# A fused attention and two-MLP kernel: its MLP products as seven block products over thirds of the tokens, with the output product between the gate's and the value's

## The chip, the cores and the metric

The kernel runs on one core of a Trainium2 chip. The metric is the device time of one execution in microseconds. The engines are TensorE (PE, matrix products, with its weight loads as PEld), VectorE (DVE), ScalarE (ACT), GpSimd (POOL) and SyncE (SP), whose queue issues the DMAs here. Each engine works through its own queue of instructions in order; semaphores hold one engine for another. PSUM, which TensorE writes, has eight banks of 512 float32 columns in each of 128 partitions.

## The reference

Windowed attention with a distance bias (4 batches of 576 tokens, 8 heads of 64, window 128), then a gated MLP, then a product of two linear maps with two more matrices. T is 2304 tokens, the model width 512.

```python
scores = where((rel >= 0) & (rel < 128), q @ k.T / 8 - slope[h] * rel, -1e9)
x = softmax(scores) @ v                                   # (2304, 512)
x = (sigmoid(x @ w_gate) * (x @ w_val)) @ w_out           # d_ff 1536
y = ((x @ w1) * (x @ w2)) @ w3 @ w_out2                   # d_ff 1024
```

## The kernel before

All products are made in three passes of float32r: every operand is split into a high part (a cast, `*_hi`) and a rest (`*_lo`, the difference), and `product` (lines 371 to 376) issues hi x hi, lo x hi and hi x lo into the same bank. So each tensor that TensorE reads costs other engines a cast and a subtraction.

**Attention.** 16 pairs of heads in 5 steps each give 80 steps; each engine has a function `slot` that works on several steps at once, with lags between scores (TensorE), `score` (VectorE, line 671), exponentials (ScalarE), `reciprocals` (VectorE, 682 and 684), `normalise` (GpSimd, 852), `turn` (TensorE), the split of the turned probabilities (ScalarE 560, VectorE 691) and `pv` (TensorE). The result is written twice: ScalarE casts it to `x_hi` (567), VectorE subtracts to `x_lo` (`out_lo`, 699). In the same slots TensorE multiplies w3 with the second output matrix (`fold`), 8 blocks in 8 steps, so that the second MLP has one matrix less; VectorE and GpSimd split w3 (646, 825).

**MLPs.** x, h and the outputs are held transposed (features in the partitions). The hidden features are taken in groups of 256: 6 groups (G1) for the first MLP, 4 (G2) for the second. In a group the tokens go by in five chunks (`CHUNKS`), four of 512 and one of 256. `stage1` makes, for a chunk and each half f of the group, the gate's bank `a_ps` and the value's bank `b_ps` from 4 blocks of x (24 matmuls a half); ScalarE makes `side` from `a_ps` (sigmoid or copy, 604), VectorE multiplies it with `b_ps` to `hid` (759), ScalarE casts `h_hi` (607) and GpSimd subtracts `h_lo` (888). `stage2` makes the four output banks `o_ps` from them, and VectorE adds each to `acc` in SBUF (769, 771). TensorE's `group` issues stage1 of the next chunk before stage2 of this one:

```python
for c in range(NCH):
    if c + 1 < NCH:
        stage1(g, c + 1, wb)
    elif more:
        stage1(g + 1, 0, 1 - wb)
    stage2(g, c, wb)
```

The next group's three weight matrices (1024 columns each) are loaded by SP (343), cast by ScalarE (597) and subtracted by GpSimd (880) once per group, into the other of two sets of buffers. At the end of the first MLP VectorE splits `acc` into the new x (780, 784). Outputs are stored from `acc` (357, 366).

## Time and profile before

| | us |
|---|---|
| median of 3 runs | 969.59 |
| the runs | 968.31, 969.59, 1548.55 |
| span of the profiled execution | 966.6 |
| TensorE busy | 937.0 |
| VectorE busy | 422.0 |
| ScalarE busy | 315.3 |
| GpSimd busy | 334.8 |

The profiled execution's own time is known as its span, from the first to the last instruction; the median of the runs is 3.0 us above it. Busy time of TensorE counts a matmul from its start to its modelled end, though the next one starts earlier, so the spacing of the starts is what a matmul costs in a row. A row of the grouped views gives a line, the engine, what is written from what, the shape and the count, then the busy time and the mean ns of one, then the engine's idle time before them and what ended it. A row of the timeline gives start and duration in us.

### The profile page before, as it was taken

What the parts mean: (1) busy time and instruction counts of PE and PEld (TensorE: products, weight loads), DVE (VectorE), ACT (ScalarE), POOL (GpSimd) and SP (SyncE); (2) the same over time, 40 slices, a digit from 0 to 9 for tenths busy, and PEclk for the clock granted to TensorE, in tenths of its full rate; (3) what the DMA queues carried; (4) which work ended last, traced back from release to release, by engine and by line L of the source; (5) the groups of instructions that cost most, each with busy time, mean ns of one, the idle gap of its engine ahead of it and who ended that gap; (6) DMA issues with size and microseconds to landing.
All of it is one profiled execution on the core that took longest, in us unless ns stands there. A gap on an engine that the chain in (4) does not pass through costs nothing.

```text
span 966.6 us, 14591 instructions
## 1 busy us (share of the span) xinstructions
PE 937.0 (97%) x4912; PEld 799.1 (83%) x4912; DVE 422.0 (44%) x1115; ACT 315.3 (33%) x819; POOL 334.8 (35%) x314
## 2 busy tenths in 40 slices
PE   5899999999999999999999999999999999999998
PEld 4788888787888888888888888888888888888887
DVE  8999999994222222232232222345322222223223
ACT  6787888774211212121222121121121111121111
POOL 7677666661331231231231241231221222322211
DMA  6333333322010010010000000000000000000022
GB/s 217 104 114 108 96 109 102 106 101 77 22 44 1 22 44 1 22 43 0 22 24 19 22 22 22 22 22 22 22 22 22 22 22 22 1 0 1 1 87 109
DMA packets 28984, 44.95 MB, mean 47 GB/s; under 512 B 2464, under 2 KB 14368, under 8 KB 28960
## 3 DMA queue, kind: packets, MB, share of 16 engines
q1 hardware_dynamic: 28960, 44.64, 14.7%
q8 instruction: 14, 0.23, 0.1%
q14 instruction: 10, 0.08, 0.0%
HBM read 37.81 MB, written 6.82 MB: 46 GB/s over the span
## 4 chain that ended last, share of the span: by engine, by line
PE 80%; DVE 13%; issue 4%; ACT 1%; DMA 0%; SPq 0%; DVEq 0%; ACTq 0%
PE a_ps L374 9%; PE o_ps L375 9%; PE a_ps L375 9%; PE o_ps L374 9%; PE b_ps L375 8%; PE b_ps L374 8%; PE o_ps L376 8%; PE b_ps L376 8%; PE a_ps L376 8%; DVE pt_lo L691 3%; DVE rowsum L682 2%; DVE x_lo L699 2%; DVE w_hi L646 2%; DVE negs L671 2%; PE pv_ps L374 1%
## 5 line engine op out<-in xcount | busy, mean ns | idle before, releaser
L888 POOL TENSOR_TENSOR h_lo<-hid,h_hi 128x512 fp32r<-128x512 f32 (+1 forms) x100 | 118.0, 1180 | 555.9 <-ACT h_hi L607 555.9
L759 DVE TENSOR_TENSOR hid<-b_ps,side 128x512 f32<-128x512 f32 (+1 forms) x100 | 63.8, 638 | 406.2 <-PE b_ps L376 404.7
L604 ACT ACTIVATE side<-a_ps 128x512 f32<-128x512 f32 (+1 forms) x100 | 55.5, 555 | 483.2 <-PE a_ps L376 483.1
L374 PE MATMUL a_ps<-x_hi,w_hi 128*128 128x512 f32 (+1 forms) x400 | 147.4, 369 | 0.3 <-DVE w_lo L748 0.3
L375 PE MATMUL o_ps<-h_lo,w_hi 128*128 128x512 f32 (+1 forms) x400 | 147.3, 368 | 0.0
L375 PE MATMUL a_ps<-x_lo,w_hi 128*128 128x512 f32 (+1 forms) x400 | 147.3, 368 | 0.0
L374 PE MATMUL o_ps<-h_hi,w_hi 128*128 128x512 f32 (+1 forms) x400 | 147.3, 368 | 0.0
L375 PE MATMUL b_ps<-x_lo,w_hi 128*128 128x512 f32 (+1 forms) x400 | 147.2, 368 | 0.0
L376 PE MATMUL b_ps<-x_hi,w_lo 128*128 128x512 f32 (+1 forms) x400 | 147.2, 368 | 0.0
L376 PE MATMUL o_ps<-h_hi,w_lo 128*128 128x512 f32 (+1 forms) x400 | 147.2, 368 | 0.0
L376 PE MATMUL a_ps<-x_hi,w_lo 128*128 128x512 f32 (+1 forms) x400 | 147.2, 368 | 0.0
L374 PE MATMUL b_ps<-x_hi,w_hi 128*128 128x512 f32 (+1 forms) x400 | 147.2, 368 | 0.0
L771 DVE TENSOR_TENSOR acc<-o_ps,acc 128x512 f32<-128x512 f32 (+1 forms) x160 | 102.1, 638 | 95.2 <-PE o_ps L376 95.0
L607 ACT CAST h_hi<-hid 128x512 fp32r<-128x512 f32 (+1 forms) x100 | 57.4, 574 | 105.7 <-DVE hid L759 105.6
L374 PEld LDWEIGHTS a_ps<-x_hi,w_hi 128*128 128x128 f32 x400 | 75.4, 189 | 13.0 <-issue 0.4
L374 PEld LDWEIGHTS o_ps<-h_hi,w_hi 128*128 128x128 f32 x400 | 75.4, 189 | 12.6
L376 PEld LDWEIGHTS a_ps<-x_hi,w_lo 128*128 128x128 f32 x400 | 75.4, 189 | 12.6
L376 PEld LDWEIGHTS o_ps<-h_hi,w_lo 128*128 128x128 f32 x400 | 75.4, 189 | 12.6
L374 PEld LDWEIGHTS b_ps<-x_hi,w_hi 128*128 128x128 f32 x400 | 75.4, 189 | 12.5
L375 PEld LDWEIGHTS o_ps<-h_lo,w_hi 128*128 128x128 f32 x400 | 75.4, 189 | 12.5
L375 PEld LDWEIGHTS b_ps<-x_lo,w_hi 128*128 128x128 f32 x400 | 75.4, 189 | 12.5
L376 PEld LDWEIGHTS b_ps<-x_hi,w_lo 128*128 128x128 f32 x400 | 75.4, 189 | 12.5
(69 smaller groups left out, 1440.9 us busy)
## 6 DMA issues: line engine op xcount, KB each, us to landing
k_raw<-kT SPq DMA_DIRECT2D x16, 288.0 KB, 2.8
q_raw<-qT SPq DMA_DIRECT2D x16, 288.0 KB, 2.8
v_raw<-v SPq DMA_DIRECT2D x16, 256.0 KB, 2.7
w_raw<-w3t SPq DMA_DIRECT2D x16, 256.0 KB, 3.1
w_raw<-w SPq DMA_DIRECT2D x8, 512.0 KB, 3.5
w_raw<-w_gate SPq DMA_DIRECT2D x6, 512.0 KB, 3.5
w_raw<-w_val SPq DMA_DIRECT2D x6, 512.0 KB, 3.5
w_raw<-w_out SPq DMA_DIRECT2D x6, 512.0 KB, 3.5
```

What stands on the lines that cost most here:

```text
L374: pe.matmul(out, lh, rh, start=start, stop=False)
L375: pe.matmul(out, lh, rl, start=False, stop=False)
L376: return pe.matmul(out, ll, rh, start=False, stop=stop)
L604: nc.scalar.activation(side[f][:, 0:n], ps_a[f][:, 0:n], func).then_inc(side_ready, 1)
L607: nc.scalar.copy(h_hi[hb][f][:, 0:n], hid[f][:, 0:n]).then_inc(h_hi_done, 1)
L646: nc.vector.tensor_copy(w3_hi[:, cols], w3_raw[:, cols]).then_inc(w3_hi_done, 1)
L671: op = nc.vector.tensor_tensor_reduce(negs[buf][:, j * KW + skip:(j + 1) * KW], pA[buf][:, first:first + KW - skip], bias[pb][:, skip:KW], ...
L682: nc.vector.tensor_scalar(rowsum2[:, cols], rowsum[:, cols], 1e-9, None, ALU.add).then_inc(sum_done, 1)
L691: nc.vector.tensor_tensor(out=cols(pt_lo[buf]), in0=cols(pB[buf]), in1=cols(pt_hi[buf]), op=ALU.subtract).then_inc(pt_split, 1)
L759: nc.vector.tensor_tensor(out=hid[f][:, 0:n], in0=ps_b[f][:, 0:n], in1=side[f][:, 0:n], op=ALU.mult).then_inc(hid_ready, 1)
L771: op = nc.vector.tensor_tensor(out=acc[:, cols], in0=ps_o[o][:, 0:size(c)], in1=acc[:, cols], op=ALU.add)
L888: nc.gpsimd.tensor_tensor(out=h_lo[hb][f][:, 0:n], in0=hid[f][:, 0:n], in1=h_hi[hb][f][:, 0:n], op=ALU.subtract).then_inc(h_split, 1)
```

## The change

The first two products of each MLP are made by a seven-product scheme on blocks of 2 x 2. The weights of a group (512 x 256) and x of some tokens (512 x 768) are cut in halves in both directions. Seven products M1 to M7 of a sum of weight blocks with a sum of x blocks, 256 x 128 by 256 x 384 each, take the place of eight block products. The tokens are taken in three passes (`NPASS`) of `TP` = 768, each through all ten groups of both MLPs; `TH` is 384.

- TensorE: `multiply(g, m, js)` makes the seven products of the gate (m = 0) or of the value (m = 1), `project(g)` the eight output tiles. Five banks hold the products (M7 is added to the bank of M4 after VectorE has read it, M6 to that of M1), three the output tiles. All loops are written out.
- ScalarE: copies M2 and M5 to `s21` and `s12`, applies the sigmoid in SBUF, casts the weights (`weights_hi`: two blocks of 512 columns in all, five sums of 1280), w_out (`out_hi`, 1024) and the hidden pieces.
- VectorE: `weight_sums` makes the five sums of weight blocks (512, 512 and 256 columns, both inputs in SBUF), `combine` makes the four quarters C21, C12, C11, C22 of the gate (in `side`) or the value (in `hid`) with six sums of 384 columns, each with one input in PSUM, `hidden` multiplies `hid` with `side`, both in SBUF, and `add_up` adds the output tiles.
- GpSimd: `weights_lo`, `out_lo` and `hidden_lo` subtract.
- Sums of x blocks (`x_sum`, 768 columns) and their splits are made before each layer of each pass, for the first in the last slots of the attention. The attention writes its result once, in float32 (`xf`), so VectorE's `out_lo` of lines 694 to 701 is gone; `xf` is overwritten by the outputs. `fold` has one block in each of 64 slots.

```diff
--- before.py
+++ after.py
-CH = 512
-CHUNKS = [slice(c, min(c + CH, T)) for c in range(0, T, CH)]
+NPASS = 3
+TP = T // NPASS
+TH = TP // 2
...
+M2, M4, M5, M3, M1, M7, M6 = range(7)
+W_S5, W_S2, W_D6, W_D7, W_S1, W_11, W_22 = range(7)
+W_OF = {M2: W_S2, M4: W_22, M5: W_S5, M3: W_11, M1: W_S1, M7: W_D7, M6: W_D6}
+BANK_OF = {M2: 0, M4: 1, M5: 2, M3: 3, M1: 4, M7: 1, M6: 4}
...
```

TensorE:

```diff
+            def multiply(g, m, js):
+                q, inst = 2 * g + m, instance(g)
+                if js[0] == M2:
+                    pe.wait_ge(wq_split[m], g + 1)
...
+                    elif j == M7:
+                        pe.wait_ge(c_done[C21], q + 1)
+                    elif j == M6:
+                        pe.wait_ge(u11_done, q + 1)
+                    for kk in range(2):
+                        w = slice(W_OF[j] * GW + kk * P, W_OF[j] * GW + (kk + 1) * P)
+                        x = slice((2 * j + kk) * TH, (2 * j + kk + 1) * TH)
+                        mm = product(quad_ps[BANK_OF[j]][:, 0:TH], (wq_hi[m][:, w], wq_lo[m][:, w]),
+                                     (xs_hi[:, x], xs_lo[:, x]),
+                                     start=kk == 0 and j not in (M7, M6), stop=kk == 1, onto=j in (M7, M6))
+                    mm.then_inc(prod_done, 1)
+            def project(g):
+                pe.wait_ge(wo_split, g + 1)
+                pe.wait_ge(h_split, 4 * (g + 1))
...
+                    wait(pe, acc_done, t - 2)
+                    for f in range(FG):
+                        w = slice(f * DM + o * P, f * DM + (o + 1) * P)
+                        hp = piece(2 * f + c)
+                        mm = product(ps_o[t % 3][:, 0:TH], (wo_hi[hb][:, w], wo_lo[hb][:, w]),
+                                     (h_hi[hb][:, hp], h_lo[hb][:, hp]), start=f == 0, stop=f == FG - 1)
+                    mm.then_inc(o_done, 1)
...
+            for g in range(NG):
+                if g == 0:
+                    multiply(0, 0, (M5, M3, M1, M7, M6))
+                else:
+                    multiply(g, 0, ALL)
+                if not first_of(g):
+                    project(g - 1)
+                multiply(g, 1, ALL)
+                if last_of(g):
+                    project(g)
-            def group(g, wb, more):
-                for c in range(NCH):
-                    if c + 1 < NCH:
-                        stage1(g, c + 1, wb)
-                    elif more:
-                        stage1(g + 1, 0, 1 - wb)
-                    stage2(g, c, wb)
```

ScalarE:

```diff
+            def weights_hi(g, m):
+                act.wait_ge(rawq_in[m], 16 * (g + 1))
+                wait(act, prod_done, 14 * g - 7 * (1 - m))
+                if g == 0:
...
+                four = raw_q[m][:, :].rearrange("p (b n) -> p b n", b=4)
+                nc.scalar.copy(wq_hi[m][:, W_11 * GW:7 * GW].rearrange("p (b n) -> p b n", b=2), four[:, 0:4:3, :]
+                               ).then_inc(wq_hi_done[m], 1)
+                act.wait_ge(wsum_done[m], 3 * (g + 1))
+                nc.scalar.copy(wq_hi[m][:, 0:5 * GW], wsum[m][:, :]).then_inc(wq_hi_done[m], 1)
...
+            for g in range(NG):
+                more = g + 1 < NG
+                keep_21(2 * g)
+                out_hi(g)
+                keep_12(2 * g)
+                sigmoid(g, C21)
+                sigmoid(g, C12)
+                keep_21(2 * g + 1)
+                sigmoid(g, C11)
+                sigmoid(g, C22)
+                keep_12(2 * g + 1)
+                if more:
+                    weights_hi(g + 1, 0)
+                for n, k in enumerate((C21, C12, C11, C22)):
+                    hidden_hi(g, n, k)
+                if more:
+                    weights_hi(g + 1, 1)
+                    if last_of(g):
+                        for j in (M2, M4, M5, M3, M1, M7, M6):
+                            xs_hi_part(instance(g) + 1, j)
```

VectorE:

```diff
+            def weight_sums(g, m):
+                dve.wait_ge(rawq_in[m], 16 * (g + 1))
+                wait(dve, wq_split[m], g)
...
+                raw, out = raw_q[m], wsum[m]
+                four = raw[:, :].rearrange("p (b n) -> p b n", b=4)
+                nc.vector.tensor_tensor(out=out[:, 0:2 * GW].rearrange("p (b n) -> p b n", b=2), in0=four[:, 0:4:2, :],
+                                        in1=four[:, 1:4:2, :], op=ALU.add).then_inc(wsum_done[m], 1)
+                nc.vector.tensor_tensor(out=out[:, 2 * GW:4 * GW], in0=raw[:, 0:2 * GW], in1=raw[:, 2 * GW:4 * GW],
+                                        op=ALU.subtract).then_inc(wsum_done[m], 1)
+                nc.vector.tensor_tensor(out=out[:, 4 * GW:5 * GW], in0=raw[:, 0:GW], in1=raw[:, 3 * GW:4 * GW],
+                                        op=ALU.add).then_inc(wsum_done[m], 1)
+            def combine(g, m):
+                q, out = 2 * g + m, (side, hid)[m]
+                if q == 0:
+                    dve.wait_ge(x_ready, NSTEP)
+                if m == 1:
+                    wait(dve, h_split, 4 * g)
+                dve.wait_ge(prod_done, 7 * q + M4 + 1)
+                dve.wait_ge(s21_done, q + 1)
+                nc.vector.tensor_tensor(out=out[:, piece(C21)], in0=quad_ps[1][:, 0:TH], in1=s21[:, :],
+                                        op=ALU.add).then_inc(c_done[C21], 1)
+                dve.wait_ge(prod_done, 7 * q + M3 + 1)
+                dve.wait_ge(s12_done, q + 1)
+                nc.vector.tensor_tensor(out=out[:, piece(C12)], in0=quad_ps[3][:, 0:TH], in1=s12[:, :],
+                                        op=ALU.add).then_inc(c_done[C12], 1)
+                wait(dve, c_done[C22], q)
+                nc.vector.tensor_tensor(out=t22[:, :], in0=quad_ps[3][:, 0:TH], in1=s21[:, :],
+                                        op=ALU.subtract).then_inc(t22_done, 1)
+                dve.wait_ge(prod_done, 7 * q + M1 + 1)
+                wait(dve, c_done[C11], q)
+                nc.vector.tensor_tensor(out=u11[:, :], in0=quad_ps[4][:, 0:TH], in1=s12[:, :],
+                                        op=ALU.subtract).then_inc(u11_done, 1)
+                if m == 1:
+                    hidden(g, 0, C21)
+                    hidden(g, 1, C12)
+                dve.wait_ge(prod_done, 7 * q + M7 + 1)
+                dve.wait_ge(u11_done, q + 1)
+                nc.vector.tensor_tensor(out=out[:, piece(C11)], in0=quad_ps[1][:, 0:TH], in1=u11[:, :],
+                                        op=ALU.add).then_inc(c_done[C11], 1)
+                dve.wait_ge(prod_done, 7 * q + M6 + 1)
+                dve.wait_ge(t22_done, q + 1)
+                nc.vector.tensor_tensor(out=out[:, piece(C22)], in0=quad_ps[4][:, 0:TH], in1=t22[:, :],
+                                        op=ALU.add).then_inc(c_done[C22], 1)
+                if m == 1:
+                    hidden(g, 2, C11)
+                    hidden(g, 3, C22)
+            def hidden(g, n, k):
+                dve.wait_ge(c_done[k], 2 * g + 2)
+                if g % GP < G1:
+                    before = 4 * (g // GP * G1 + g % GP)
+                    dve.wait_ge(sig_done, before + n + 1)
+                nc.vector.tensor_tensor(out=hid[:, piece(k)], in0=hid[:, piece(k)], in1=side[:, piece(k)],
+                                        op=ALU.mult).then_inc(hid_done, 1)
...
+            for g in range(NG):
+                more = g + 1 < NG
+                combine(g, 0)
+                if more:
+                    weight_sums(g + 1, 0)
+                if not first_of(g):
+                    add_up(g - 1)
+                combine(g, 1)
+                if more:
+                    weight_sums(g + 1, 1)
+                if last_of(g):
+                    inst = instance(g) + 1
+                    if g % GP == GP - 1:
+                        if more:
+                            for j in (M4, M3, M1, M6):
+                                x_sum(inst, j)
+                        add_up(g)
...
+                        add_up(g, range(4))
+                        x_lo_part(inst, M2)
+                        x_sum(inst, M4)
+                        add_up(g, (4, 5))
+                        x_lo_part(inst, M4)
+                        add_up(g, (6, 7))
+                        x_sum(inst, M3)
+                        x_sum(inst, M1)
+                        x_lo_part(inst, M3)
+                        x_sum(inst, M6)
+                        x_lo_part(inst, M1)
+                        x_lo_part(inst, M6)
-            def out_lo(t, s):
...
-                    op = nc.vector.tensor_tensor(out=out_cols(x_lo, t, s - 1, h), in0=pv_cols(pC[buf], i, h),
-                                                 in1=out_cols(x_hi, t, s - 1, h), op=ALU.subtract)
```

GpSimd:

```diff
+            def weights_lo(g, m):
+                pool.wait_ge(wq_hi_done[m], 2 * g + 1)
+                four = raw_q[m][:, :].rearrange("p (b n) -> p b n", b=4)
+                cols = slice(W_11 * GW, 7 * GW)
+                pool.wait_ge(wsum_done[m], 3 * (g + 1))
+                nc.gpsimd.tensor_tensor(out=wq_lo[m][:, cols].rearrange("p (b n) -> p b n", b=2),
+                                        in0=four[:, 0:4:3, :],
+                                        in1=wq_hi[m][:, cols].rearrange("p (b n) -> p b n", b=2), op=ALU.subtract)
+                pool.wait_ge(wq_hi_done[m], 2 * g + 2)
+                nc.gpsimd.tensor_tensor(out=wq_lo[m][:, 0:5 * GW], in0=wsum[m][:, :], in1=wq_hi[m][:, 0:5 * GW],
+                                        op=ALU.subtract).then_inc(wq_split[m], 1)
...
+            for g in range(NG):
+                more = g + 1 < NG
+                out_lo(g)
+                if more:
+                    weights_lo(g + 1, 0)
+                for n, k in enumerate((C21, C12, C11, C22)):
+                    hidden_lo(g, n, k)
+                if more:
+                    weights_lo(g + 1, 1)
+                    if last_of(g):
+                        inst = instance(g) + 1
+                        x_lo_part(inst, M5)
+                        x_sum(inst, M7)
+                        x_lo_part(inst, M7)
```

How the queues stand. ScalarE, one stretch of the MLPs before (the last MLP, where `a_ps0` and `a_ps1` are the gate's banks of the two halves), with the same stretch of work in other chunks left out:

```order
L604 ACTIVATE side0<-a_ps0 128x512
L604 ACTIVATE side1<-a_ps1 128x512
L607 CAST h_hi10<-hid0 128x512
L607 CAST h_hi11<-hid1 128x512
L597 CAST w_hi1<-w_raw 128x1024
```

And ScalarE after, one whole group of the first MLP (`quad_ps0` holds M2, `quad_ps2` M5, `wq` the gate's or value's weights):

```order
L631 COPY s21<-quad_ps0 128x384
L623 CAST wo_hi1<-raw_o 128x1024
L637 COPY s12<-quad_ps2 128x384
L643 ACTIVATE side<-side 128x384 x2
L631 COPY s21<-quad_ps0 128x384
L643 ACTIVATE side<-side 128x384 x2
L637 COPY s12<-quad_ps2 128x384
L612 CAST wq_hi0<-raw_q0 128x512
L615 CAST wq_hi0<-wsum0 128x1280
L650 CAST h_hi1<-hid 128x384 x4
L612 CAST wq_hi1<-raw_q1 128x512
L615 CAST wq_hi1<-wsum1 128x1280
```

The next group's gate weights now stand behind the copy of the value's M5, and the next group's first copy of M2 behind all hidden pieces and the value's weights. GpSimd before, one stretch of the last group but one:

```order
L888 TENSOR_TENSOR h_lo<-hid,h_hi 128x512 x4
L880 TENSOR_TENSOR w_lo<-w_raw,w_hi 128x1024
L888 TENSOR_TENSOR h_lo<-hid,h_hi 128x512 x2
L880 TENSOR_TENSOR w_lo<-w_raw,w_hi 128x1024
L888 TENSOR_TENSOR h_lo<-hid,h_hi 128x512 x2
L880 TENSOR_TENSOR w_lo<-w_raw,w_hi 128x1024
```

And GpSimd after, one whole group (`quad` weights `wq`, first the next gate's, then the next value's):

```order
L1020 TENSOR_TENSOR wo_lo<-raw_o,wo_hi 128x1024
L1010 TENSOR_TENSOR wq_lo<-raw_q,wq_hi 128x512
L1014 TENSOR_TENSOR wq_lo<-wsum,wq_hi 128x1280
L1026 TENSOR_TENSOR h_lo<-hid,h_hi 128x384 x4
L1010 TENSOR_TENSOR wq_lo<-raw_q,wq_hi 128x512
L1014 TENSOR_TENSOR wq_lo<-wsum,wq_hi 128x1280
```

Before, two pieces of h_lo stood between two weight subtractions; now the gate's weights stand ahead of all four hidden pieces. VectorE before, at the end of the first MLP:

```order
L759 TENSOR_TENSOR hid<-b_ps,side 128x512 x2
L771 TENSOR_TENSOR acc<-o_ps,acc 128x512 x4
L780 CAST x_hi<-acc 128x512 x4
L784 TENSOR_TENSOR x_lo<-acc,x_hi 128x512 x4
L759 TENSOR_TENSOR hid<-b_ps,side 128x256 x2
```

And VectorE after, in a middle group from the value's t22 on:

```order
L820 TENSOR_TENSOR t22<-quad_ps3,s21 128x384
L824 TENSOR_TENSOR u11<-quad_ps4,s12 128x384
L847 TENSOR_TENSOR hid<-hid,side 128x384 x2
L831 TENSOR_TENSOR hid<-quad_ps1,u11 128x384
L835 TENSOR_TENSOR hid<-quad_ps4,t22 128x384
L847 TENSOR_TENSOR hid<-hid,side 128x384 x2
L797 TENSOR_TENSOR wsum1<-raw_q1 128x512
L799 TENSOR_TENSOR wsum1<-raw_q1 128x512
L801 TENSOR_TENSOR wsum1<-raw_q1 128x256
L813 TENSOR_TENSOR side<-quad_ps1,s21 128x384
```

Two multiplications of `hidden` now stand ahead of the sum that reads M7's bank (line 831), and both inputs of `hidden` are in SBUF.

## Rows read from the trace of the kernel before

**Rows 1.** The page: its first line and the chain that ended last

```profile
span 966.6 us, 14591 instructions
...
PE 80%; DVE 13%; issue 4%; ACT 1%; DMA 0%; SPq 0%; DVEq 0%; ACTq 0%
```

**Rows 2.** Stretches: length, then busy us of PE, PEld, DVE, ACT, POOL (x count), clock, DMA

```profile
50.00:100.00 50.00, 46.23 (x314) 40.29 (x313) 47.71 (x180) 40.28 (x137) 35.88 (x44) 1.00 0.35 105
```

**Rows 3.** Tile views: ns min/median/max, first and last start in us; then TensorE alone

```profile
L374 PE MATMUL a_ps<-x_hi,w_hi x400: 277/389/473, 223.4 to 953.7; 128*128 128x512 f32 x107, 128*128 128x256 f32 x27
...
L376 PE MATMUL o_ps<-h_hi,w_lo x400: 279/389/390, 246.5 to 963.7; 128*128 128x512 f32 x107, 128*128 128x256 f32 x27
...
225.00:963.00 738.00, 738.00 (x3595) 1.00 0.08 25
```

**Rows 4.** Timeline of TensorE, starts of matmuls in a row

```profile
306.19 0.28 PE L374 MATMUL o_ps<-h_hi,w_hi 128*128 128x256 f32 x1
...
309.07 0.40 PE L374 MATMUL a_ps<-x_hi,w_hi 128*128 128x512 f32 x1
...
312.49 0.39 PE L374 MATMUL b_ps<-x_hi,w_hi 128*128 128x512 f32 x1
...
318.61 0.39 PE L374 MATMUL b_ps<-x_hi,w_hi 128*128 128x512 f32 x1
```

**Rows 5.** Groups by line and shape: busy us, mean ns, idle before

```profile
L888 POOL TENSOR_TENSOR h_lo<-hid,h_hi 128x512 fp32r<-128x512 f32 x80 | 103.3, 1292 | 490.4 <-ACT h_hi L607 490.4
...
L771 DVE TENSOR_TENSOR acc<-o_ps,acc 128x512 f32<-128x512 f32 x128 | 88.5, 691 | 87.9 <-PE o_ps L376 87.9
...
L880 POOL TENSOR_TENSOR w_lo<-w_raw,w_hi 128x1024 fp32r<-128x1024 f32 x27 | 65.0, 2406 | 0.0
...
L607 ACT CAST h_hi<-hid 128x512 fp32r<-128x512 f32 x80 | 49.3, 617 | 93.6 <-DVE hid L759 93.6
...
L597 ACT CAST w_hi<-w_raw 128x1024 fp32r<-128x1024 f32 x30 | 31.5, 1050 | 0.0
...
L771 DVE TENSOR_TENSOR acc<-o_ps,acc 128x256 f32<-128x256 f32 x32 | 13.6, 425 | 7.3 <-PE o_ps L376 7.1
```

**Rows 6.** Timeline of all engines at the first chunk

```profile
233.11 0.61 ACT L607 CAST h_hi<-hid 128x512 fp32r<-128x512 f32 x1
...
233.80 1.29 POOL L888 TENSOR_TENSOR h_lo<-hid,h_hi 128x512 fp32r<-128x512 f32 x1 [14.08 <-ACT h_hi L607]
...
234.91 0.39 PE L376 MATMUL b_ps<-x_hi,w_lo 128*128 128x512 f32 x1
...
235.33 0.69 DVE L759 TENSOR_TENSOR hid<-b_ps,side 128x512 f32<-128x512 f32 x1 [2.34 <-PE b_ps L376]
```

**Rows 7.** Timelines of VectorE and GpSimd in the attention; line 646 alone

```profile
10.11 2.17 DVE L737 TENSOR_TENSOR wo_lo<-wo_raw,wo_hi 128x512 fp32r<-128x512 f32 x1
...
10.46 1.26 POOL L825 TENSOR_TENSOR w_lo<-w_raw,w_hi 128x512 fp32r<-128x512 f32 x1
...
129.47 1.31 DVE L646 CAST w_hi<-w_raw 128x512 fp32r<-128x512 f32 x1
...
129.68 0.82 POOL L852 TENSOR_TENSOR prob<-exps,recip 128x384 f32<-128x384 f32 x1
...
L646 DVE CAST w_hi<-w_raw x16: 475/1308/1316, 9.3 to 208.0; 128x512 fp32r<-128x512 f32 x16
```

**Rows 8.** Groups by line of VectorE, 20 to 215 us

```profile
L699 DVE TENSOR_TENSOR x_lo<-pv_ps,x_hi 64x128 f32 (+2 forms) x146 | 39.9, 273 | 1.0
```

**Rows 9.** Timeline of TensorE at the start

```profile
8.88 0.41 PE L374 MATMUL score_ps<-k_hi,q_hi 128*128 128x256 f32 x1
...
9.95 0.41 PE L376 MATMUL score_ps<-k_hi,q_lo 128*128 128x256 f32 x1
...
16.27 0.41 PE L375 MATMUL score_ps<-k_lo,q_hi 128*128 128x256 f32 x1
```

**Rows 10.** The page: DMA issues, KB each, us to landing

```profile
w_raw<-w_gate SPq DMA_DIRECT2D x6, 512.0 KB, 3.5
```

886 lines of the change are left out of this document (440 added, 446 removed).

## The prediction

> **What bounds the kernel now.** I read the page first: the span is 966.6 us and the chain that ended last is 80% TensorE and 13% VectorE [rows 1]. Then the table by stretches: from 225 to 963 us TensorE is busy all the time, while before that, as in 50 to 100 us, VectorE is the fullest (47.71 of 50), with TensorE at 46.23 and ScalarE at 40.28 [rows 2]. So there are two parts: the attention, up to the first MLP matmul at 223.4 us, held by VectorE's queue, and the two MLPs, held by TensorE alone, whose last matmul starts at 963.7 [rows 3].
>
> TensorE's price, from starts of rows in a line: 27 steps of 512 columns take 318.61 - 312.49 = 6.12 us, 0.227 each; 24 of 256 columns take 309.07 - 306.19 = 2.88 us, 0.120 each [rows 4]. By the line between them 384 columns cost 0.1735. The MLP is 2880 matmuls of 512 and 720 of 256: 652.9 + 86.4 = 739.3 us, and 223.4 to 963.8 is 740.4: nothing waits.
>
> **What the change takes from TensorE.** A group now has 2 x 7 products of 6 matmuls and 8 output tiles of 6, all of 384 columns: 132 a group, 30 groups, 3960 x 0.1735 = 687.1 us. That is 52.2 us less, if TensorE never waits. A product or a tile is 1.04 us, the gate's seven (G) 7.29, the output projection (O) 8.33, the value's seven (V) 7.29; a group would be 22.9.
>
> **What it adds around it.** Prices at the new shapes by straight lines through rows 5: VectorE 384 columns 0.56 (0.48 from start to start in a row); ScalarE 384 columns 0.51 and 1280 columns 1.27 (0.617 + 768 x 0.433/512), 0.1 less from start to start; GpSimd 384 columns 1.01, 512 columns 1.29, 1280 columns 2.96. Handing over: VectorE starts 0.42 us after the start of the last 512-column matmul (234.91 to 235.33), so 0.19 after its slot ends; a ScalarE result is taken by GpSimd 0.08 later (233.72 to 233.80) [rows 6].
>
> GpSimd now has 6144 columns a group (two weight splits of 512 + 1280, w_out 1024, hidden 4 x 384): 14.5 us. That fits into 22.9. The order does not fit. And there is the port that VectorE and GpSimd have in common. At 10.11 us a VectorE subtraction with both inputs in SBUF took 2.17 us, where 512 columns take 0.69 [rows 5]. GpSimd's operation from 10.46 to 11.72 ran meanwhile, and VectorE ended 0.56 after it. The cast of line 646 takes 475 ns at best and 1308 at the median; the one of 129.47 ends at 130.78, 0.28 after the GpSimd operation that ran until 130.50 [rows 7]. So such a VectorE operation waits out GpSimd's operation, and the next one too if that is ready. In the MLPs of before no VectorE operation overlaps GpSimd with two SBUF inputs (hid reads PSUM). Now ten do in a group: 4 of `hidden`, 6 of `weight_sums`.
>
> The Trainium skill (SBUF — State Buffer, "Who interferes with whom") says the same of a two-input operation against GpSimd's reads, and that the loser fully blocks. This trace agrees, with 2.17 us against 0.69; the skill adds that it needs no fast mode, which is what makes `hidden` and `weight_sums` suspects.
>
> **One group, followed through the queues.** Let v be the start of V of group g-1 (times from v).
> 1. The value's M5 is visible at 3.31. ScalarE's keep_12, queued ahead of the next gate weights, runs until 3.80; weights_hi first part to 4.32, second to 5.49. GpSimd's weights_lo: 4.40 to 5.69, and 5.65 to 8.61. Only then may G of group g start: 8.7 to 8.8 with its first weight load, where V ended at 7.29. Lost: 1.5.
> 2. VectorE reaches hidden(C21) at 5.87, inside GpSimd's 5.65 to 8.61: it ends at 9.1, hidden(C12) at 9.5, C11 at 10.0. M4 needs that bank: 10.2 instead of 9.8. Lost: 0.4.
> 3. GpSimd takes the two hidden pieces 9.76 to 11.74, back to back, so hidden(C11) waits to 11.74, hidden(C22) ends at 12.65, and the value's weight_sums share the port with two more pieces: they end at 14.1 or, if GpSimd comes in between, 16.1. ScalarE's second split waits for them (15.5 or 17.4), and keep_21 of G stands behind it: 15.9 or 17.8. C21 follows at 16.6 or 18.5; M7 needs it, due at 14.4. Lost: 2.3 or 4.2.
> 4. ScalarE's out_hi (1.05) stands ahead of keep_12, then C12, t22, u11 in a row: M6 starts at 19.0 or 21.0 instead of 17.8 or 19.7. Lost: 1.2. G ends at 20.1 or 22.0.
> 5. The next weight_sums meet GpSimd's weights_lo and out_lo until 22.7, so add_up starts at 24.2: O's fourth tile waits 1.7 in the early case, hardly in the late one. O ends at 30.1 or 30.3.
> SP's loads are no limit: each 512 KB lands in 3.5 us [rows 10], and its buffer is free some ten us before the data are wanted. So both arbitrations give about 30.2 us a group, against 22.9 without a wait and 24.8 if the port cost nothing (steps 1 and a little of 4 remain). This goes for the 24 groups with O between.
>
> **Ends of layers.** After the last group of a layer, O must wait for the hidden pieces, which stand behind the next weights: it starts at 15.3, not 7.3. Inside a pass (3 times) x is then split: xs M5, the M7 sum and its split on GpSimd and eight VectorE operations of 768 columns (0.95, GpSimd 1.85), with the port between them; M3 starts at 30.8, M1 at 34.5, G ends at 38.4. At a pass change (twice) four sums stand ahead of add_up and wait for about 7 us of GpSimd: add_up starts at 27.4, G ends at 42.3. Without the port both are about 30. The last group: O ends at 19.3. The first G adds 7.3.
>
> **Attention.** It loses the x_lo copies, 39.9 us of VectorE between 20 and 215 [rows 8]. TensorE's own work there is 864 matmuls of up to 256 columns at 0.120, 192 of 512 at 0.227 and 256 transposes, at most 0.12 each: 178 us of 223, so at most 45 come back; I take 20, because ScalarE and the hand-overs follow close. It gains at its end 9 VectorE operations of 0.95, 6 weight sums (3.1), three GpSimd operations of 1.85 and four of the weight splits (8.5): between 0 (hidden) and 25; I take 11. G starts at 223.4 - 9 = 214; bounds 190 to 225.
>
> **The clock.** In the first microseconds TensorE's 256 columns take 1.07/5 = 0.214 us, its lower level (1.2 GHz; the page's granted column says 1.00 there), and so until about 16.5 [rows 9]; about 6.7 us of matmuls at half speed, 3.3 lost. That followed 7.5 us of idleness. The five ends of layers have gaps of that size; between 0 and 3.3 each, I take the nearest row, 3.3: 16.5.
>
> The Trainium skill (TensorE: Matmul & The Clock Gate, "Why this matters for your kernels") warns that idle gaps between bursts bring the lower clock back; no row of this trace shows the clock fall after it had risen. By that rule step 3's late case may be reached as well, which is the third rival's time.
>
> **The sum.** 214 + 7.3 + 24 x 30.2 + 3 x 38.4 + 2 x 42.3 + 19.3 = 1165.2; with 16.5 of clock 1181.7; from the last matmul to the end 2.9 (2.7 now) gives a span of 1184.6; the median of the runs, 969.6, is 3.0 over the profiled span, so 1188 us.
>
> **Rivals.**
> - The port costs little: GpSimd's operations leave gaps and VectorE slips in. Against it stand rows 7; for it, that they are of the attention alone. 214 + 7.3 + 24 x 24.8 + 5 x 30 + 19.3 + 5.9 = 992 us. Chance 0.14.
> - Not slower: TensorE never runs dry within a group. This is decided in step 1, if from M5's end to the split weights takes under the 4.2 us of the four products left, not 5.5: all 24 groups at 22.9 give 946 us. It would need GpSimd to split 1792 columns in under 2.7 us; rows 5 price them at 4.2. Chance 0.04.
> - The clock falls inside the groups too: step 3's gap of up to 4.2 us is the longest. One loss of 3.3 in each of 24 groups: 1267 us. For it, rows 9; against it, that gaps of 1 us in the attention do nothing. Chance 0.12.
> - The forecast: 0.70. Its own bounds: a group between 28 and 32 (48 us either way), the ends of layers 40 less, the attention 24 less or 11 more.
>
> **The numbers.** The first two rivals lie below the range; it takes in the third. Faster by over 2%, about what a measurement of this kernel can tell, comes only from the second rival: 0.03. Within 2%: the rest of it and the lower edge of the first, 0.04. Slower: 0.93.
>
> **What would show it.** In the profile of the changed kernel: matmul spacing 0.17 us within products; about 25% idle TensorE in the MLPs, waiting for wq_lo on GpSimd before M2, for VectorE's C21 before M7 and for u11 before M6; the mean of its line 847 (`hidden`) far over 0.55 us, and of 797 to 801 (`weight_sums`) over 0.7; G to G about 30 us. If line 847 stays near 0.55 the port story is wrong and the first rival holds. If GpSimd's wq_lo of 1280 columns is well under 2.9 us, step 1 is wrong. If matmuls in the groups take twice the spacing, the third rival holds.

## The result and the profile after

The changed kernel takes 1232.27 us (median of 4 runs, 1231.83 to 1233.2) beside 969.04 for the kernel before on the same chip: a ratio of 1.272, 95% interval 1.270 to 1.274. One of the four executions of the kernel before took 1548.55 us and is not in the ratio. The forecast was 1188, in a range of 1080 to 1270. So the sign, the range and the waits of the seven products held, and the size was 44 us short. Two of its terms were wrong all the same: the clock inside the groups and the attention. That the sum stayed near is in part luck, as the section on the reasons shows.

From the profile page of the changed kernel (first line, busy time, granted clock in 40 slices, the chain that ended last):

```profile
span 1230.2 us, 15386 instructions
...
PE 994.5 (81%) x5272; PEld 932.1 (76%) x5272; DVE 876.0 (71%) x1566; ACT 485.8 (39%) x1091; POOL 676.7 (55%) x475
...
PEclk8999987899888888988998888889799988878988
...
PE 48%; DVE 25%; issue 18%; ACT 6%; POOL 1%; DMA 1%; SPq 0%; DVEq 0%; ACTq 0%; POOLq 0%
```

Against [rows 1] TensorE's share of the chain fell from 80% to 48% and VectorE's rose from 13% to 25%. TensorE's granted clock is no longer 1.00 throughout; the mean is 0.897.

What TensorE waited for, from the waits of the changed kernel (us in total, times, longest):

```profile
PE quad_ps L410 <- DVE side L813: 85.6, 27, 3.5
PE o_ps L410 <- issue: 40.3, 6, 7.2
PE quad_ps L410 <- POOL wq_lo L1014: 28.4, 24, 1.2
PE o_ps L410 <- DVE xf L860: 10.8, 2, 5.4
PE quad_ps L410 <- DVE xs_lo L786: 9.8, 6, 2.9
PE quad_ps L410 <- DVE u L824: 8.2, 11, 0.9
```

The first row is M7 waiting for the gate's C21, in 27 of the 30 groups; the third is M2 waiting for the split weights (step 1 of the forecast), the last M6 waiting for u11 (step 4). The rows of `o_ps` and `xs_lo` are the ends of layers. Before, the MLPs had no wait at all [rows 3].

The groups of instructions that answer to [rows 5], and the two that are new on VectorE (busy us, mean ns of one):

```profile
L799 DVE TENSOR_TENSOR wsum<-raw_q 128x512 f32<-128x512 f32 x60 | 67.2, 1120 | 0.0
...
L1014 POOL TENSOR_TENSOR wq_lo<-wsum,wq_hi 128x1280 fp32r<-128x1280 f32 x60 | 177.3, 2955 | 0.0
L1026 POOL TENSOR_TENSOR h_lo<-hid,h_hi 128x384 fp32r<-128x384 f32 x120 | 149.5, 1275 | 47.5 <-ACT h_hi L650 47.5
...
L847 DVE TENSOR_TENSOR hid<-hid,side 128x384 f32<-128x384 f32 x120 | 165.1, 1415 | 0.0
```

`hidden` takes 1415 ns where 0.56 us was the price without GpSimd, the 512-column weight sums of this line 1120 where 0.69 us was. The mean of `hidden` hides a spread: 543 ns at least, 733 in the middle, 3119 at most. GpSimd's 1280 columns take 2.955 us, as forecast (2.96). Its hidden pieces, priced at 1.01, take 1.275 in the mean and 0.98 at least.

One middle group in the timeline (start us, duration us; the value's products V start at v = 344.46). Rows of TensorE, and some of ScalarE, GpSimd and VectorE, are left out between the rows shown:

```profile
350.12 2.93 POOL L1014 TENSOR_TENSOR wq_lo<-wsum,wq_hi 128x1280 fp32r<-128x1280 f32 x1
350.34 3.58 DVE L847 TENSOR_TENSOR hid<-hid,side 128x384 f32<-128x384 f32 x2
353.85 0.55 DVE L831 TENSOR_TENSOR hid<-quad_ps,u 128x384 f32<-128x384 f32 x1
354.08 5.02 POOL L1026 TENSOR_TENSOR h_lo<-hid,h_hi 128x384 fp32r<-128x384 f32 x4 [1.04 <-ACT h_hi L650]
354.78 2.03 DVE L847 TENSOR_TENSOR hid<-hid,side 128x384 f32<-128x384 f32 x2
356.73 1.50 DVE L797 TENSOR_TENSOR wsum<-raw_q 128x512 f32<-128x512 f32 x1
358.15 1.50 DVE L799 TENSOR_TENSOR wsum<-raw_q 128x512 f32<-128x512 f32 x1
359.57 0.41 DVE L801 TENSOR_TENSOR wsum<-raw_q 128x256 f32<-128x256 f32 x1
360.02 1.26 ACT L615 CAST wq_hi<-wsum 128x1280 fp32r<-128x1280 f32 x1 [2.14 <-DVE wsum L801]
361.18 0.47 ACT L631 COPY s<-quad_ps 128x384 f32<-128x384 f32 x1
361.36 2.93 POOL L1014 TENSOR_TENSOR wq_lo<-wsum,wq_hi 128x1280 fp32r<-128x1280 f32 x1
361.76 0.56 DVE L813 TENSOR_TENSOR side<-quad_ps,s 128x384 f32<-128x384 f32 x1 [1.77 <-ACT s L631]
...
363.08 0.56 DVE L817 TENSOR_TENSOR side<-quad_ps,s 128x384 f32<-128x384 f32 x1 [0.77 <-ACT s L637]
```

The reader is to see the chain of steps 2 and 3: the first two `hidden` operations stand beside GpSimd's 2.93 us and end 0.9 us after it; the weight sums take 1.50 beside GpSimd's pieces; ScalarE's cast of the weight sums waits for VectorE, and the copy of M2 (L631) stands behind that cast, so that C21 (L813) starts at 361.76, v + 17.3, though M4, the later of the two products it needs, had started at 354.45. Note the last rows too: L813 and L817 run while GpSimd reads (361.36 to 364.29) and take 0.56 each, since one of their inputs is in PSUM.

TensorE's side of the same group, two of its rows after a wait and two of the rows behind the second one:

```profile
353.09 0.44 PE L410 MATMUL quad_ps<-xs_hi,wq_hi 128*128 128x384 f32 x1 [1.18 <-POOL wq_lo L1014]
...
362.37 0.69 PE L410 MATMUL quad_ps<-xs_hi,wq_hi 128*128 128x384 f32 x1 [3.49 <-DVE side L813]
...
363.49 0.52 PE L410 MATMUL quad_ps<-xs_hi,wq_hi 128*128 128x384 f32 x1
363.81 0.52 PE L411 MATMUL quad_ps<-xs_lo,wq_hi 128*128 128x384 f32 x1
```

After the wait of 3.49 us the starts are 0.32 apart, where 0.1735 is the full rate. The table by stretches of the changed kernel shows the same as a granted clock (last three columns: clock, DMA share, GB/s):

```profile
350.00:360.00 10.00, 7.67 (x41) 6.70 (x40) 9.99 (x10) 2.53 (x5) 8.06 (x6) 1.00 0.17 52
360.00:370.00 10.00, 7.63 (x26) 7.16 (x27) 5.26 (x11) 3.91 (x6) 6.48 (x3) 0.66 0.32 106
370.00:380.00 10.00, 10.00 (x60) 10.00 (x59) 4.37 (x8) 2.05 (x5) 0.00 (x0) 1.00 0.01 2
```

0.66 over ten microseconds is a mixture of the two levels, 2.4 and 1.2 GHz. TensorE's starts show the lower one in every one of the 24 groups with an output product between: behind M7's wait, in some only behind M6, between 5 and 17 spacings are 0.32. This is the third rival's mechanism, which the forecast gave a chance of 0.12. The first row also shows VectorE busy for 9.99 of 10 us while C21 is due.

From one w_out split on GpSimd (L1020) to the next, the groups in the middle of a layer take 30.2, 30.4, 32.2 and 31.5 us (starts 271.42, 301.63, 332.07, 364.22, 395.69) and in the second MLP 31.2 and 31.0; the mean is 31.1. A pass is 331.1 us (578.22 to 909.30). The first MLP product starts at 242.6.

### The profile page after: what moved, and what is told of

It reads as the page before. It is cut to its first block, busy times and chain, and to the rows that moved or that the text cites. A ratio compares the mean times of both kernels' runs of the same rounds, so it can differ in the third digit from the quotient of the medians.

```text
span 1230.2 us, 15386 instructions
## 1 busy us (share of the span) xinstructions
PE 994.5 (81%) x5272; PEld 932.1 (76%) x5272; DVE 876.0 (71%) x1566; ACT 485.8 (39%) x1091; POOL 676.7 (55%) x475
## 4 chain that ended last, share of the span: by engine, by line
PE 48%; DVE 25%; issue 18%; ACT 6%; POOL 1%; DMA 1%; SPq 0%; DVEq 0%; ACTq 0%; POOLq 0%
PE quad_ps L410 8%; PE o_ps L410 7%; PE o_ps L411 7%; PE o_ps L412 7%; PE quad_ps L411 6%; PE quad_ps L412 6%; DVE hid L847 5%; DVE wsum L797 3%; DVE wsum L799 3%; DVE rowsum L741 2%; DVE t L820 2%; ACT exps L572 2%; ACT wo_hi L623 1%; ACT s L631 1%; DVE u L824 1%
## 5 line engine op out<-in xcount | busy, mean ns | idle before, releaser
L410 PE MATMUL quad_ps<-xs_hi,wq_hi 128*128 128x384 f32 x840 | 313.0, 373 | 135.9 <-DVE side L813 85.6
L410 PEld LDWEIGHTS quad_ps<-xs_hi,wq_hi 128*128 128x128 f32 x840 | 168.9, 201 | 174.8 <-DVE side L813 91.0
L411 PE MATMUL quad_ps<-xs_lo,wq_hi 128*128 128x384 f32 x840 | 298.9, 356 | 0.0
L412 PE MATMUL quad_ps<-xs_hi,wq_lo 128*128 128x384 f32 x840 | 298.7, 356 | 0.0
L410 PE MATMUL o_ps<-h_hi,wo_hi 128*128 128x384 f32 x480 | 177.3, 369 | 51.1 <-issue 40.3
L1014 POOL TENSOR_TENSOR wq_lo<-wsum,wq_hi 128x1280 fp32r<-128x1280 f32 x60 | 177.3, 2955 | 0.0
L1026 POOL TENSOR_TENSOR h_lo<-hid,h_hi 128x384 fp32r<-128x384 f32 x120 | 149.5, 1275 | 47.5 <-ACT h_hi L650 47.5
L411 PE MATMUL o_ps<-h_lo,wo_hi 128*128 128x384 f32 x480 | 174.3, 363 | 0.0
L412 PE MATMUL o_ps<-h_hi,wo_lo 128*128 128x384 f32 x480 | 173.6, 362 | 0.0
L411 PEld LDWEIGHTS quad_ps<-xs_lo,wq_hi 128*128 128x128 f32 x840 | 171.4, 204 | 0.0
L412 PEld LDWEIGHTS quad_ps<-xs_hi,wq_lo 128*128 128x128 f32 x840 | 171.1, 204 | 0.0
L631 ACT COPY s<-quad_ps 128x384 f32<-128x384 f32 x60 | 28.6, 476 | 358.8 <-PE quad_ps L412 358.7
L847 DVE TENSOR_TENSOR hid<-hid,side 128x384 f32<-128x384 f32 x120 | 165.1, 1415 | 0.0
L1020 POOL TENSOR_TENSOR wo_lo<-raw_o,wo_hi 128x1024 fp32r<-128x1024 f32 x30 | 74.2, 2474 | 22.1 <-ACT wo_hi L623 22.1
```

The costliest lines, as they stand in the source:

```text
L410: pe.matmul(out, lh, rh, start=start, stop=False, skip_group_check=onto)
L411: pe.matmul(out, lh, rl, start=False, stop=False, skip_group_check=onto)
L412: return pe.matmul(out, ll, rh, start=False, stop=stop, skip_group_check=onto)
L847: nc.vector.tensor_tensor(out=hid[:, piece(k)], in0=hid[:, piece(k)], in1=side[:, piece(k)], op=ALU.mult).then_inc(hid_done, 1)
L1014: nc.gpsimd.tensor_tensor(out=wq_lo[m][:, 0:5 * GW], in0=wsum[m][:, :], in1=wq_hi[m][:, 0:5 * GW], op=ALU.subtract).then_inc(wq_split[m], 1)
L1020: nc.gpsimd.tensor_tensor(out=wo_lo[g % 2][:, :], in0=raw_o[:, :], in1=wo_hi[g % 2][:, :], op=ALU.subtract).then_inc(wo_split, 1)
```

## The experiments

Every experiment but `sched_fill` is a single execution; the kernel before, taken beside each, lay between 968.3 and 969.4 us, the four of the changed kernel within 1.4 us of each other and the four of `sched_fill` within 9.6, so differences of a few us are not read as effects. Groups are timed from one w_out cast on ScalarE, or one w_out split on GpSimd, to the next. Line numbers of an experiment can differ by a few from those of the changed kernel.

**Is it the port?** In `port_free` GpSimd keeps its place in every queue, but its splits of the weights, of w_out and of the hidden pieces only write zeros and read nothing (so the rests are missing from the products; its three x operations at an end of a layer stay):

```diff
-                nc.gpsimd.tensor_tensor(out=h_lo[g % 2][:, piece(k)], in0=hid[:, piece(k)],
-                                        in1=h_hi[g % 2][:, piece(k)], op=ALU.subtract).then_inc(h_split, 1)
+                fill(h_lo[g % 2], k * TH, 384).then_inc(h_split, 1)
```

(`fill` is a row of memsets of 64 columns), and so for the weights and w_out.

> In the MLPs GpSimd's four kinds of subtraction (rests of the weights, of w_out and of the hidden pieces) are left out; in their place stand memsets of 64 columns that fill the same tiles with zeros, as many as take about the same time. So the queues, their order and GpSimd's share of the work stay, but GpSimd reads nothing from SBUF. The port theory (a VectorE operation with two SBUF inputs waits out GpSimd's reads): hidden goes from 1.4 us to 0.55, weight_sums to 0.69, a group from about 31 us to 25, the ends of layers lose 6 to 10 us each: 1040 us, between 1000 and 1080. The rival (the queues' order alone, the port costs nothing): no change, 1220 us or more.

Measured: 1024.95 us, clock 0.972; a group takes 24.63 us (ScalarE's w_out cast at 309.92 and at 334.55), against "24.8 if the port cost nothing" in the forecast. From its groups and its waits:

```profile
L847 DVE TENSOR_TENSOR hid<-hid,side 128x384 f32<-128x384 f32 x120 | 60.9, 549 | 0.0
L799 DVE TENSOR_TENSOR wsum<-raw_q 128x512 f32<-128x512 f32 x60 | 41.0, 683 | 0.0
```

```profile
PE quad_ps L410 <- DVE u L824: 22.4, 24, 0.9
```

The operations are at 549 and 683 ns, the prices read from [rows 5], and the waits for C21 (but 2.5 us in 3) and for the split weights are gone; the small wait of M6 that the forecast kept (step 4) stays. One caveat: GpSimd's fill is much shorter than the subtraction (20 memsets of 64 columns take 1.80 us, the subtraction 2.93), and in a middle group GpSimd is busy for 8.6 us where it was busy for 15.7. So the 1.2 us of step 1 went with the shorter fill and not with the port, and the other 3.8 of the 5.0 us that a group loses against `keep_warm2` below (29.63 to 24.63) are the port's as an estimate. That GpSimd's speed by itself does not hold the groups is shown by `sched_only` below, where it is busy for 15.4 us of a group of 22.9.

**Which operation's lateness costs?** Three kernels move one thing each. `early_gate` casts the next gate's weights ahead of both copies of the value:

```diff
+                if more:
+                    weights_hi(g + 1, 0)
                 keep_21(2 * g + 1)
...
                 keep_12(2 * g + 1)
-                if more:
-                    weights_hi(g + 1, 0)
```

> ScalarE's weights_hi(g + 1, 0) is moved ahead of keep_21(2g + 1), so that the next gate's weights are split while TensorE is in the output projection; nothing else moves. My walk through the queues: the wait before M2 (1.2 us a group) and the one before M4 go, hidden(C21) no longer meets GpSimd's 1280 columns, but hidden(C11) and the weight sums still meet the hidden pieces and M7 still waits over 3 us for C21, so a group takes 28 to 29 us: 1165 to 1190 us. If all the loss hung on the late gate weights, a group would fall under 25 us: under 1090 us.

1172.21 us, as the forecast's steps had it and not the rival's: M2's wait is gone, `hidden` is down to 774 ns (it now meets GpSimd less), and C21 remains:

```profile
PE quad_ps L410 <- DVE side L813: 69.4, 27, 3.3
...
PE quad_ps L410 <- DVE u L824: 18.0, 24, 0.9
```

A group takes about 29 us (267.16, 296.22, 326.05, 354.72, 384.31), though the weight sums are still at 1120 ns.

`late_value` puts ScalarE's cast of the value's weights behind the gate's copies, so that C21 no longer stands behind it:

```diff
                 keep_12(2 * g)
+                if g and not first_of(g):
+                    weights_hi(g, 1)
...
-                if more:
-                    weights_hi(g + 1, 1)
-                    if last_of(g):
+                if more and last_of(g):
+                        weights_hi(g + 1, 1)
```

> ScalarE's weights_hi(g + 1, 1) is moved behind keep_12 of the next group's gate (in the last group of a layer it stays), so that keep_21 of the gate no longer stands behind it. My walk: M7's wait for C21 shrinks from 3.5 to about 1.5 us, but GpSimd's split of these weights and of w_out then runs into the time of the next weight_sums, add_up starts late and TensorE waits there instead: no gain in sum, 1210 to 1240 us. The rival (keep_21 behind the value's weights is the cause by itself): M7's wait of 85.6 us in all goes and does not come back: 1150 us or less.

1206.03, four below my range and far from the rival's. C21's wait halved and came back as a wait of the output tiles for `add_up` (52.3 us in all, 10.8 before the move), which is step 5's wait in another place:

```profile
PE quad_ps L410 <- DVE side L814: 40.9, 27, 1.6
...
PE o_ps L410 <- DVE xf L861: 39.3, 19, 4.8
...
PE o_ps L410 <- DVE xf L859: 13.0, 6, 2.2
```

The granted clock rose from 0.897 to 0.929, which I had not put in; whether the four microseconds below the range are the clock was not tested.

`hidden_last` moves the two first `hidden` operations behind C22:

```diff
-                if m == 1:
-                    hidden(g, 0, C21)
-                    hidden(g, 1, C12)
...
                 if m == 1:
+                    hidden(g, 0, C21)
+                    hidden(g, 1, C12)
                     hidden(g, 2, C11)
```

> In VectorE's combine of the value all four hidden come behind C11 and C22. My walk: only the wait before M4 (about 0.2 us a group) goes, M7 is still held by keep_21: 1215 to 1235 us. If hidden ahead of C11 were what delays the next gate: a loss of 2 us or more a group comes back, under 1180 us.

1223.98, within the range: step 2's part is small (8 us in all, by one execution), and the wait for C21 stays 85.6 us although `hidden` falls to 867 ns. None of the three moves gives back more than 60 of the 263 us. So no one operation's place costs the time by itself, and a shorter `hidden` brings little as long as C21 is late for another reason.

**What does the clock cost?** `keep_warm` fills part of the wait before M7 with twelve matmuls whose result is overwritten:

```diff
                     elif j == M7:
+                        if m == 0 and g and not first_of(g):
+                            wait(pe, acc_done, 8 * (g - 1))
+                            for k in range(12):
+                                pe.matmul(ps_o[8 * (g - 1) % 3][:, 0:TH], wq_hi[m][:, 0:P], xs_hi[:, 0:TH],
+                                          start=True, stop=True)
                         pe.wait_ge(c_done[C21], q + 1)
```

> The changed kernel, with 12 more matmuls of 384 columns ahead of M7 of the gate in the 24 groups that wait there over 3 us for C21. Their result goes into an output bank that the next tile overwrites, so nothing that is computed changes. They fill 2.1 us of the wait and leave some 1.4. The clock theory (after such a wait TensorE works about 6 us at its lower level and loses 1 to 3 us a group): 1165 to 1205 us, the mean granted clock above 0.95. The rival (the loss is all waiting, the lower clock is hidden in it): 1225 to 1235 us; and if the added matmuls cost their own time, 1240 or more.

1218.28, outside the expected range and above it: 14 us back. Its groups show why. Some take 29.6 us (300.52 to 330.15), others 31.2 (330.15 to 361.34); the second kind, 16 of the 24, has a fall of the clock, now mostly behind M6, whose wait is 0.91 us. Stretches of `keep_warm`:

```profile
300.00:330.00 30.00, 26.11 (x144) 24.82 (x144) 21.12 (x32) 10.31 (x18) 16.09 (x10) 1.00 0.16 53
330.00:360.00 30.00, 26.88 (x141) 25.92 (x142) 19.74 (x29) 8.99 (x17) 14.49 (x10) 0.94 0.16 53
```

So both waits, before M7 and before M6, had to be filled. `keep_warm2` has 17 such matmuls before M7 and 5 before M6.

> The changed kernel with 17 extra matmuls of 384 columns ahead of the gate's M7 and 5 ahead of its M6 in the 24 groups with an output product between (their results are overwritten). In keep_warm (12 before M7 alone) the groups whose 10 us stretches all show a granted clock of 1.00 took 29.63 us from one w_out split to the next, those with a stretch of 0.83 took 31.2; the fall came after the 0.91 us wait for u11 before M6. If the clock is what costs, filling both waits (3.5 and 0.9 us) leaves every group at 29.6 to 29.8 and no stretch of a group below 1.00: 1218 less about 16 x 1.5, so 1190 to 1205 us. Rival: the difference of 1.5 us is due to something else than the clock (the gap before M2 and VectorE's queue), or the clock falls at another gap (1.2 us before M2): groups stay at 31 and the time at 1213 to 1225.

1192.06 us, as the clock theory has it. Two of its stretches, each as long as a group:

```profile
300.00:330.00 30.00, 28.18 (x158) 26.90 (x157) 21.13 (x32) 10.08 (x18) 16.12 (x10) 1.00 0.16 53
330.00:360.00 30.00, 28.21 (x158) 26.93 (x157) 21.13 (x32) 10.23 (x18) 16.12 (x10) 1.00 0.17 54
```

Every group in the middle of a layer now takes 29.6 us, and no start in the 24 groups shows the lower level. VectorE's, ScalarE's and GpSimd's work and queues are unchanged (`hidden` 1414 ns). The clock inside the groups therefore costs 1232.3 - 1192.1 = 40 us, about 24 x (31.1 - 29.63) = 35 by the middle groups; its falls at the ends of layers are still there and are not in this figure. The price in a group is 1.5 us and not the 3.3 to 3.4 that a stretch of 0.66 takes from TensorE. Many falls are shorter (from 5 spacings on), and without the fall M6 waits for u11 again: 22.4 us in 24 groups in `keep_warm` beside 8.2 in 11 in the changed kernel.

**The attention.** `att_only` spreads its new work: the seven parts of x from slot 50 in every third slot, the weight sums at slots 72 and 80 with their splits one slot later, and their DMAs issued at slot 68 instead of after the last slot.

```diff
-PREP_SLOT = 74
+XS_AT = {50 + 3 * j: j for j in range(7)}
+PREPS = (72, 80)
```

> Only the attention part of the changed kernel is altered: the seven sums and splits of the first x are spread over slots 50, 53 ... 68 instead of 62 to 68, the first weights are loaded at slot 68 instead of after the last slot, and their sums and splits stand at slots 72/73 and 80/81 instead of 74/75 and 76/77. My reading (the attention lost its 19 us by x sums in seven slots in a row, 14 us, and by the 6 us for which VectorE waits for the load): the first MLP product starts at 225 to 230 us instead of 242.6: 1215 to 1221 us. The rival (the fold in every slot and the lower clock hold it): under 5 us, 1228 to 1232.

1223.34, 9 us back and between the two. `att_thin` leaves the place and cuts the size instead: it does the attention's x work on 64 columns and zeroes the rest at the start, so its first pass leaves out most of x.

> The changed kernel with the first x operations of the attention's slots (VectorE's sums and subtractions, ScalarE's casts, GpSimd's sum and subtractions for the seven products of the first pass) on 64 columns in place of 768; the rest of those tensors is zeroed at the program's start, so the first pass computes with a cut x. The weight splits and all of the MLPs stay. Measured is the stretch from the start of the 57th reciprocal (before the x work begins) to the first MLP product: before 162.2 to 223.4, 61.2 us; changed 157.0 to 242.6, 85.6 us. If the x work in seven slots in a row is what costs, the stretch falls to 65 to 72 us (what stays above 61 being the weight splits and VectorE's 6.0 us wait for their DMA); the time is then 1212 to 1222 with some 5 us of zeroing at the start. Rival: the loss is of something else (the DMA wait, the weight splits): 80 us or more, and 1228 to 1238.

The stretch from the 57th reciprocal (160.2) to the first MLP product (234.6) is 74.4 us, again between the two, and the time 1225.76 (its slot loop starts 3.0 us later). So of the 24.4 us by which that stretch grew (61.2 to 85.6), 11.2 are the size of the x work, and the other 13.2 stay. The reciprocals divide them further. From the 57th to the 65th, the slots with the x work, it is 21.0 us before, 35.3 in the changed kernel and 23.6 in `att_thin`: 14.3 more, of which 2.6 stay. From the 65th to the first MLP product it is 40.2, 50.3 and 50.8: 10 us more with none of VectorE's x work in them, where the weight sums and splits stand and VectorE waits for their DMA. Waits of VectorE in `att_thin`, 157 to 243 us:

```profile
DVE wsum L801 <- DMA raw_q<-w_gate: 5.8, 1, 5.8
```

Two of the slots there took 8.6 and 6.7 us instead of 2.2 to 2.9. How the 10 us divide between that wait and the operations was not separated.

**Does the order alone do it?** `sched_only` keeps all operations, and so the port, and changes the queues. ScalarE casts the next gate's weights in two parts around `keep_21` of the value, and the value's behind `keep_12` of the gate, ahead of `out_hi`. VectorE takes the weight sums after `add_up`, and GpSimd follows. TensorE's first four output tiles wait for three hidden pieces instead of four.

```diff
+                if g and not first_of(g):
+                    weights_hi(g, 1)
                 out_hi(g)
...
+                if more:
+                    weights_hi_a(g + 1, 0)
                 keep_21(2 * g + 1)
...
+                if more:
+                    weights_hi_b(g + 1, 0)
                 keep_12(2 * g + 1)
```

> Queue order alone, nothing left out: ScalarE splits the next gate's weights while TensorE is in the output projection and the next value's weights in the next gate's time; out_hi stands behind keep_12; VectorE's weight_sums (both) stand behind add_up; the output projection's first four tiles wait for three hidden pieces. The sums and splits of x at the ends of layers stay as they are. My walk: no wait of TensorE within a group, 22.9 to 23.5 us a group, the clock stays at its upper level, the ends of layers still 34 to 38 us: 990 to 1020 us. If the port (GpSimd and VectorE still need 20 of 23 us on it) were a limit whatever the order: a group over 26 us, over 1070 us.

1038.65 us: 19 above the range, 31 below the rival's. The middle groups of a layer are at 22.9 us (starts 294.08, 316.99, 339.95, 362.88), which is 132 x 0.1735: TensorE does not wait there. `hidden` still takes 958 ns, and no product in those groups waits for it:

```profile
L864 DVE TENSOR_TENSOR hid<-hid,side 128x384 f32<-128x384 f32 x120 | 110.4, 958 | 0.0
```

The contention is less than in the changed kernel (1415 ns there, 549 without GpSimd's reads), but it has not gone. What the expectation underrated is everything else: the second interval of the first MLP at 24.9, the intervals across an end of a layer at 38.4 and 39.7 us, the one behind the first of them at 25.1, and the attention.

`sched_x` gives VectorE all sums and splits of x at the ends of layers, GpSimd's too, interleaves them with `add_up` and puts M6's split behind the first C21; `sched_all` adds the spread attention. `sched_fill` moves the output product of the group before the last one of a layer behind that one's value products, so that TensorE has something to do while the last hidden pieces come; the next weights are split behind those pieces there. The diff shows TensorE's part.

```diff
-                if not first_of(g):
+                if not first_of(g) and not last_of(g):
                     project(g - 1)
                 multiply(g, 1, ALL)
                 if last_of(g):
+                    project(g - 1)
                     project(g)
```

> As the run before, and at the ends of layers all twelve sums and rests of x are VectorE's (0.9 us each, where GpSimd takes 1.85), ordered as the seven products need them, and M6's stand behind the first C21. My walk: an end of a layer takes 27 to 29 us, five times: 955 to 975 us. If GpSimd's share did not matter: within 10 us of the run before.

> The queue order, the x sums and the attention of the three runs before together. Sum of the parts: 15 us less than the run with the x sums: 940 to 960 us, so level with or faster than the kernel before (969). If the parts share one cause, it is not under 960.

> The best version so far, and in the last group of a layer the output projection of the group before stands behind the value's products instead of ahead of them, so that it fills the wait for the hidden pieces; the weights of the next group are split behind the hidden pieces there. Six waits of 3.9 us and the lower clock behind them go, while the gate's and the value's products now follow each other and some of C21 comes late: 15 to 25 us less than 1024, so 999 to 1009 us. The rival (the hidden pieces only wait at another place, for VectorE and the port): within 6 us of 1024. In neither case is it under the 969 of the kernel before.

Measured 1026.71, 1023.76 and 1019.88 (the last one a median of 4, 1011.45 to 1021.08; ratio 1.050, interval 1.0455 to 1.0546). The first two missed their ranges by 52 and 64 us: I had worked out the end of a layer as if its waits went away, and each of them moved. TensorE's waits in `sched_fill`:

```profile
PE quad_ps L421 <- DVE side L843: 22.2, 12, 2.7
PE quad_ps L421 <- DVE xs_lo L816: 21.0, 13, 3.3
PE o_ps L421 <- DVE xf L892: 11.0, 10, 1.1
```

The six waits of `o_ps` for the hidden pieces, 22.7 us in `sched_all`, are gone. But the waits for C21 grew from 15.6 to 22.2, those for `xs_lo` from 15.1 to 21.0, and 11.0 us of waits for `add_up` came new, together 23.5 us. Of the 15 to 25 us expected, four came, which is less than the spread of its own four executions. So the rival of this expectation, that the wait only moves, is what happened. `sched_fill` has the lowest time of all versions of the change, still 5% slower than before: in no order that was tried did the seven products win.

## Why the forecast came out as it did

Times from v are those of the group shown above.

**TensorE's work.** 384 columns were priced at 0.1735 us; 39 matmuls from 344.46 to 351.23 take 6.77, 0.1736 each. Right.

**Step 1**, the weights' split: GpSimd's 1280 columns at v + 5.66 (forecast 5.65), G at v + 8.63 (8.7), lost 1.2 in all 24 groups. Right, and `early_gate` takes it away.

**Step 2**: the two `hidden` operations at v + 5.88, M4 at v + 10.0 (10.2). Right; `hidden_last` gives it 8 us.

**Step 3**: of the two arbitrations the trace shows mostly the late one's mechanism, GpSimd coming between VectorE's operations (1.50 instead of 0.69), and C21 comes at v + 17.3, between the 16.6 and 18.5 of the two. GpSimd's hidden pieces were priced at 1.01 and take 1.275. The loss without the clock is read from `keep_warm2` and `port_free`: 29.63 against 24.63 a group. The forecast had 30.2 against 24.8, so 5.4 instead of 5.0. That agreement is closer than it deserves. The forecast's 24.8 still held the 1.5 us of step 1, which `port_free` does not have; its 24.63 is 22.9 and the waits and restarts before M7, M6 and M4. By the estimate above the port itself is 3.8 us a group. Over the kernel those two differ by 167 us, 120 of them in the 24 groups.

The Trainium skill's rule used in the forecast (SBUF — State Buffer, "Who interferes with whom"), a two-input operation against GpSimd's reads, holds in both directions here: 1415 ns becomes 549 when GpSimd's splits read nothing, and the operations with an input in PSUM stay at 0.56 beside it.

**Step 4** was put at 1.2 in every group; M6's wait is 0.9 in every group where the clock stays up, and is hidden by the slower matmuls where it fell. Right in kind. **Step 5**: `add_up` hardly waits in the late case; right, and it is what takes over in `late_value`.

**The clock** is the first step that failed. I charged 3.3 us at five ends of layers (16.5) and gave falls inside the groups a chance of 0.12, at 3.3 each. They occur in all 24 groups, after the wait before M7 or the one before M6 that follows it, and cost 1.5 each: 40 us in all. The reason given against it, that gaps of 1 us in the attention do nothing, said nothing on the gap of up to 4.2 us that step 3 itself forecast. The Trainium skill (TensorE: Matmul & The Clock Gate, "Why this matters for your kernels") had warned of it; by that rule the trace agrees: 1.00 before the wait of 3.49 us, 0.66 in the stretch after it.

Since a group without the clock was forecast 0.6 too long (30.2 for 29.63), the two partly cancel: 31.1 a group. That is luck, as is that a fall cost less than half of the 3.3 at which the third rival had it: at that price the measured time would have been about 24 x 1.8 = 43 us longer by estimate, 1275, above the range. Per pass, which holds two ends of layers, the forecast had 322.3 and 6.6 of clock, 328.9, and 331.1 was measured. The ends of layers were near: 46.41 + 25.04 us for the interval across the end and the one after it, against 38.4 + 30.2, and 48.85 + 24.32 at a pass change against 42.3 + 30.2. The MLPs in all: 1230.2 - 242.6 = 987.6, forecast 1184.6 - 214 = 970.6, 17 more.

**The attention** is the second step that failed, and it leaves the larger part of what the sum lacks: "G starts at 214", bounds 190 to 225; it starts at 242.6, outside them. Two terms were wrong. The removed x_lo copies were to bring 20 us; up to the 57th reciprocal they brought 162.20 - 157.04 = 5.2, although that slot loop started 1.9 later, so 7.1. TensorE is then what holds it, as the stretch of the changed kernel shows (span, PE busy):

```profile
100.00:125.00 25.00, 24.84 (x181) 23.14 (x181) 21.28 (x84) 22.33 (x78) 21.21 (x24) 1.00 0.42 128
```

I had bounded the gain by TensorE's work at full pace over the whole attention (45 us) and taken a value between, where the table of [rows 2] already had it at 46.23 of 50. And the added work was to cost 11 (at most 25); the stretch after the 57th reciprocal grew by 24.4. I had added up the operations' durations (9 x 0.95 and so on) as if any of them could slip beside the slots. They stood in seven slots in a row, in chains from VectorE to ScalarE to VectorE, ahead of every engine's next slot: eight slots took 35.3 us instead of 21.0. The other 10 us came behind them, with the weight sums and splits; the wait for the weights' DMA, 6.0 us of VectorE in the changed kernel, was put at nothing in the forecast. Together 7.1 - 1.9 - 24.4 = -19.2, the 19 us from 223.4 to 242.6.

So the 45.6 us by which the span exceeds the forecast are 28.6 of attention and 17 of MLP. The first rival (the port costs little, 992) fell with `port_free`; the second (not slower) with every wait of step 1.

Where the whole 263 us come from, by the kernels: about 40 are the clock inside the groups; 167 more go when GpSimd's splits read nothing (and take little over half of their time, as said, which by the estimate of 1.2 us a group is some 29 of them); of the remaining 56 (1025 to 969) 16 are in the attention (first product at 239.6 in `port_free`, 223.4 before) and 40 in the MLPs, where TensorE's saving of 52 us is more than used up by 1.7 us in each of 24 groups and by the ends of layers. `sched_only` shows that the port's part needs the queue order too: with GpSimd reading as before and another order, 194 of the 263 us are gone.

## What to carry to other kernels

A scheme with fewer products moves work to the engines that make its operands, and its products depend on each other through them. Follow one period through each queue, and charge every VectorE operation with two SBUF inputs with GpSimd's operation that stands beside it, but look first for an order in which nobody waits for those operations: with GpSimd reading, the middle groups took 31.1 us in one order and 22.9 in another. Work that is added to a pipelined loop can cost more than its own durations (nine operations of 0.95 us and what hangs on them cost 14.3 us here), and if a wait like the 3.5 us of M7 is forecast in a period of a TensorE-bound stage, the clock behind it is to be priced in every period.

## What the runs showed of the hardware that was not expected

- After a wait of 3.49 us TensorE runs at the lower level, 0.32 us per matmul of 384 columns where 0.1735 is the rate. In `keep_warm` waits of 1.4 and then 0.9 us, whose ends are 2.3 us apart, were followed by it in 16 of the 24 groups, and in 8 not. In `sched_all` a wait of 3.89 us had it behind it (0.79 in 374 to 382 us), one of 2.72 had not (1.00 in 390 to 400). So the length of one wait alone did not decide it. One of the two waits in `keep_warm` that were followed by it:

```profile
330.52 0.69 PE L410 MATMUL quad_ps<-xs_hi,wq_hi 128*128 128x384 f32 x1 [0.91 <-DVE u L829]
...
331.33 0.52 PE L412 MATMUL quad_ps<-xs_hi,wq_lo 128*128 128x384 f32 x1
```

- The falls of the clock, of which a stretch of 0.66 takes 3.4 us from TensorE, cost a group 1.5 us in the mean.
- GpSimd's operations too are longer beside VectorE's: its hidden pieces take 0.98 us at least and 1.275 in the mean, and at an end of a layer, where both read SBUF, the same is seen. From the timeline of the changed kernel, GpSimd:

```profile
432.70 1.84 POOL L1001 TENSOR_TENSOR xs_lo<-xf,xs_hi 128x768 fp32r<-128x768 f32 x1 [5.89 <-ACT xs_hi L603]
...
439.58 2.56 POOL L1001 TENSOR_TENSOR xs_lo<-xsum,xs_hi 128x768 fp32r<-128x768 f32 x1 [2.55 <-ACT xs_hi L603]
442.10 3.08 POOL L1020 TENSOR_TENSOR wo_lo<-raw_o,wo_hi 128x1024 fp32r<-128x1024 f32 x1
```

VectorE in the same microseconds:

```profile
435.28 2.57 DVE L777 TENSOR_TENSOR xsum<-xf 128x768 f32<-128x768 f32 x1
...
439.51 3.45 DVE L786 TENSOR_TENSOR xs_lo<-xsum,xs_hi 128x768 fp32r<-128x768 f32 x2
```

The same shape takes GpSimd 1.84 us and 2.56, and the 1024 columns 3.08 where 2.37 is usual; VectorE's two subtractions of two inputs in SBUF, 0.95 each alone, overlap both. That was not varied, so the cause is argued from these rows.
